# The reciprocal of a softmax's row sums issued one step later, and two subtractions of half a tile made one, in a hand-ordered attention pipeline

## The reference

```python
# q, k, v: (2, 8, 768, 64); centroids: (8, 16, 64)
q_assign = argmax(q_n @ c_n.T); k_assign = argmax(k_n @ c_n.T)
mask = q_assign[..., :, None] == k_assign[..., None, :]
scores = where(mask, scale * q @ k.T, -1e9)
attn = exp(scores - max(scores))
attn = attn / (sum(attn) + 1e-9)
x = (attn @ v)                      # as 1536 rows of 512
x = ((x @ w1) * (x @ w2)) @ w3 @ w_out
h = x @ w_in
out = (maximum(h, 0) + alpha * minimum(h, 0)) @ w_out2
```

## Time and profile before

| | |
|---|---|
| median of 3 runs | 774.82 us (771.75 to 774.99) |
| the profiled execution, its own time | 772.69 us |
| its span, first to last instruction | 770.9 us |
| mean granted TensorE clock | 0.998 |
| PE busy, PE weight loads busy | 750.2 us (97%), 644.9 us (84%) |
| DVE, ACT, POOL busy | 415.4 us (54%), 317.3 us (41%), 154.2 us (20%) |
| attention steps with turned tiles | from 74 to 317 us of the span |

### The profile page before, as it was taken

How to read it: one execution, slowest core, us unless ns; L and a number is a source line. 1 busy time by engine, 2 the same in 40 slices (tenths; PEclk the granted TensorE clock), 3 DMA queues, 4 the chain that set the end, 5 groups by cost and what they waited for, 6 DMA issues and landing times.

```text
span 770.9 us, 10682 instructions
## 1 busy us (share of the span) xinstructions
PE 750.2 (97%) x3810; PEld 644.9 (84%) x3810; DVE 415.4 (54%) x636; ACT 317.3 (41%) x627; POOL 154.2 (20%) x195
## 2 busy tenths in 40 slices
PE   5999999999999999899999999999999999999998
PEld 4888898898898897788888888888888888888886
DVE  4425989998899896642211153276333443434342
ACT  4325887888888786532211142242112101020112
POOL 2040544855747643210000000000000000000000
PEclk9999999999999999999999999999999999999999
DMA  9545375576666433320000021231000000010001
GB/s 293 159 111 132 75 166 123 124 157 134 133 140 143 95 77 86 102 83 1 0 1 1 0 82 57 80 102 63 0 1 33 23 1 1 1 54 1 1 0 55
DMA packets 64859, 55.74 MB, mean 72 GB/s; under 512 B 31520, under 2 KB 53040, under 8 KB 64816
## 3 DMA queue, kind: packets, MB, share of 16 engines
q1 hardware_dynamic: 64816, 55.16, 28.2%
HBM read 31.50 MB, written 3.19 MB: 45 GB/s over the span
## 4 chain that ended last, share of the span: by engine, by line
PE 76%; POOL 12%; issue 7%; DVE 3%; ACT 1%; POOLq 1%; DVEq 0%; ACTq 0%
PE slot L600 55%; PE acc L600 16%; PE slot L665 3%; POOL oh L510 1%; POOL v L484 1%; POOL v L480 1%; POOL c L502 1%; POOL c L503 1%; POOL xf L533 1%; PE acc L613 1%; DVE pl L1171 1%; DVE nm L1165 1%; PE slot L713 1%; POOL c L500 1%; POOL c L508 1%
## 5 line engine op out<-in xcount | busy, mean ns | idle before, releaser
L600 PE MATMUL slot<-xh,w 128*128 128x512 f32 x768 | 247.8, 389 | 0.0
L600 PEld LDWEIGHTS slot<-xh,w 128*128 128x128 f32 x768 | 144.3, 188 | 29.9
L600 PE MATMUL slot<-xl,w 128*128 128x512 f32 x384 | 149.5, 389 | 0.0
L1065 ACT CAST gh<-gf 128x512 fp32r<-128x512 f32 x48 | 29.9, 623 | 203.2 <-PE acc L600 186.0
L1165 DVE TENSOR_REDUCE nm<-slot 128x1 f32<-128x768 f32 x96 | 90.9, 947 | 19.3 <-PE slot L600 18.6
L1171 DVE TENSOR_TENSOR pl<-slot,ph 128x384 fp32r<-128x384 f32 x192 | 97.3, 547 | 5.8 <-ACT ph L939 5.5
L939 ACT CAST ph<-slot 128x384 fp32r<-128x384 f32 x192 | 83.7, 488 | 36.2 <-PE slot L665 35.8
L931 ACT ACTIVATE pf<-slot,nm 128x768 f32<-128x768 f32 x96 | 87.8, 915 | 14.6 <-DVE nm L1165 14.3
L665 PE MATMUL slot<-ident,pf 128*128 128x128 f32 x576 | 81.9, 276 | 6.8 <-DVE pl L1171 6.7
L600 PEld LDWEIGHTS slot<-xl,w 128*128 128x128 f32 x384 | 72.1, 188 | 14.9
L600 PE MATMUL slot<-k,q 96*128 96x384 f32 (+1 forms) x384 | 83.1, 337 | 0.0
(11 more groups left out here) (115 smaller groups left out, 1004.2 us busy)
## 6 DMA issues: line engine op xcount, KB each, us to landing
stage<-in_moe_w SPq DMA_DIRECT2D x16, 256.0 KB, 3.3
stage<-in_moe_w_in SPq DMA_DIRECT2D x16, 256.0 KB, 2.8
stage<-in_moe_w_out SPq DMA_DIRECT2D x16, 256.0 KB, 3.0
stage<-in_moe_w SPq DMA_DIRECT2D x6, 512.0 KB, 4.4
qk<-in_q SPq DMA_DIRECT2D x16, 192.0 KB, 4.0
qk<-in_k SPq DMA_DIRECT2D x16, 192.0 KB, 4.1
vn<-in_v SPq DMA_DIRECT2D x16, 192.0 KB, 4.1
q<-k SPq DMA_DIRECT2D x16, 192.0 KB, 3.7
```

What stands on the lines that cost most here:

```text
L600: return nc.tensor.matmul(o, a, b, start=start, stop=stop)
L1065: copy(gh[j % 2][:, :], gf[j % 2][:, :]).then_inc(gh_done, 1)
```

## The change

Two things are edited. The reciprocal (DVE), the write of its row and its spreading (SP) each go one step later (lags 2, 3, 4 become 3, 4, 5). And in the steps with m = 10, 11, 0, 1, 2, 3 the low part of the turned tile is one operation over both banks, 128x768, which waits for both high parts and then raises `pl_done` by two; in the other six steps it stays two operations of 128x384. The choice goes by m alone, so it also holds from step 82 on, where these steps have no operand work. Of 192 operations of 128x384, 96 become 48 of 128x768.

```diff
+OPERAND_STEPS = (10, 11, 0, 1, 2, 3)
...
-                j = inverted_now(c, last, 3)
+                j = inverted_now(c, last, 4)
                 if j is not None:
                     inverse_row(it, j)
-                j = inverted_now(c, last, 4)
+                j = inverted_now(c, last, 5)
                 if j is not None:
                     inverse_spread(it, j)
...
             def probabilities_lo(it, g):
+                if (g + LT) % 12 in OPERAND_STEPS:
+                    dve.wait_ge(ph_done, 2 * tile(it, g) + 2)
+                    tt_(pl[g % NPH][:, :, :], wide(turned_p), f32(ph[g % NPH][:, :, :]), ALU.subtract
+                        ).then_inc(pl_done, 2)
+                    return
                 for b in range(2):
                     dve.wait_ge(ph_done, 2 * tile(it, g) + b + 1)
                     tt_(pl[g % NPH][:, b, :], turned_p[:, b, 0:HS], f32(ph[g % NPH][:, b, :]), ALU.subtract
...
-                j = inverted_now(c, last, 2)
+                j = inverted_now(c, last, 3)
                 if j is not None:
                     inverse(it, j)
```

## The result

The changed kernel takes 774.50 us (median of 22 runs, 773.64 to 776.75), the kernel before 772.76 (22 runs). The ratio is 1.0021, 95% interval 1.0013 to 1.0029: slower by 1.6 us (1.0 to 2.2). That is inside the 0.5% called no change, but the sum had -0.2: small as it is, the difference goes the other way. That it came so near hides a step that failed, a loss that was not in the sum, and a gain that was not in it either. The profiled execution takes 774.49, of which its span is 772.7, against 772.69 and 770.9 before.

A forecast was written before the change was run, and what follows sets the result against it. PE, busy for 97% of the span, was taken as the bound. Gain 2.83 against losses 1.59 and 1.05 gave -0.2 us: 772.5 for the profiled execution, 774.6 as median; 80% range 769.5 to 779.5.

The forecast's parts named there:

- The reciprocal's stall goes: DVE's wait for POOL's row sums ends, so step 10's transposes lose their 1.04 us delay; T9 to T11 become 5.03.
- The rival in which the reciprocal still holds DVE: On DVE, the wait for POOL moves along to the pick: slower, 782.2 us; chance 0.05.
- The single low part's own time: DVE's 128x768 low-part operation takes 0.953 us, and 1.01 from its start to the released transposes.
- rival "dear": DVE's single low part costs 1.094 us, 0.14 more at 32 places: up to 780.6 us; chance 0.16.
- The ring: Turn to turn through the one buffer of turned tiles: 0.64 + 0.89 + 1.01 = 2.54 us, above PE's 2.39 with operand work.
- T81 to T88: Transposes of steps 81 to 88: 16.14 us becomes 17.73, from 5.03 and five turns of 2.54; loss 1.59.
- T94 to T97: Transposes of steps 94 to 97: 0.41 from later release and 0.64 from one longer turn; loss 1.05 us.
- The step that failed: SP's row write and spreading one step later were costed at nothing, since their readers come three steps later.
- The six periods: Transposes of m = 9 to m = 2, six times: 78.73 us becomes 75.90, 12.65 each; gain 2.83.
- The net: Whole kernel: -2.83 + 1.59 + 1.05 = -0.2 us, no change within 0.5%.
- The first rival: The single low part delays nothing and the reciprocal's gain stays: 8.6 us faster, 766.2 us; chance 0.09.
- The third rival: Reciprocal still holds DVE: 3.9 us lost in six periods, 2.5 in steps 82 to 88, 1.05 behind; 782.2; chance 0.05.

The follow-up runs named there:

- The splits: Against later reciprocal, masks first, two low-part operations: in six steps, either the first waits for both high parts (767.16 us) or both banks release at the end (768.36).
- the second experiment: Only the single low parts, against the kernel before; reciprocal, row and spreading stay at their old places: 780.72 us, ratio 1.0098.

## Why the prediction was right or wrong

- **The reciprocal's stall goes: right.** No wait is left at the reciprocal, T10 is not late, and T9 to T11 are 5.00 (5.03 forecast). The rival in which the reciprocal still holds DVE is refuted.
- **The single low part's own time: right.** 0.955 us for 0.953, and 1.01 from start to release. The rival "dear" is refuted; nothing about the operation is dear. DVE lost no time by it, two operations held it 0.93 and one 0.87 us.
- **The ring: right as a mechanism, mis-sized by 0.02 to 0.14.** The term for "its reader starts behind the pair of high parts" was 0.89, read where a reader had started 0.03 behind a single one; it measured 0.96, 0.10 behind the end. That belongs to the single operation: two operations that wait for both high parts start 0.03 behind, as had been read. In the last steps two turns of five start 1.07 behind the low part instead of 1.01. That makes the loss of T81 to T88 2.06 where 1.59 stood. The splits show that it takes both halves, the wait and the late release, to make the ring the bound.
- **T94 to T97: right** as far as it can be told. 0.89 lost, 1.05 forecast, in a stretch that moves by 0.4 from profile to profile. The ring in it is 2.62 where 2.54 was worked out.
- **The step that failed: "I cost these at nothing", on SP.** The sentence looked at the transfers that move and their readers. It did not look at the queue's other end: when DVE and PE get earlier by the 1.04 us of T10, a wait which had just been covered comes to light. The masks of the next pair stand in SP's queue behind a transfer that waits for POOL, and POOL had not become earlier. It takes 1.34 us of this change's 2.83, and 2.4 us (2.9 in medians) from what the later reciprocal alone could bring. The question that the prediction asked for DVE, what is late next, was not put to SP and PE's scores.
- **The six periods.** Of 2.83, 0.97 came; 1.34 went to the masks, 0.5 to rings of 2.62 and 2.68 in the last two periods. The 0.74 given back from T14 to T15 was not in the sum: the first step with cluster products is 2.97 to 3.00 long where it was 3.09 to 3.12, each time behind a step in which PE's loads had waited. No run tests why.
- **Not in the sum at all:** +0.9 us ahead of step 4, with the clock at 0.50 for 3 us; not shown to belong to the change.
- **The net.** -0.2 was forecast, +1.8 is in the profiles: +1.9 of missing gain, +0.4 more loss from T81 to T89, +0.9 ahead of step 4, against -0.7 given back at T15, -0.2 from T94 to T97 and -0.2 elsewhere. The range held it. That the net is small in both is a cancelling, not a confirmation of each term: 3.1 us of unforeseen loss stood against 1.1 of unforeseen gain. And that the forecast of 774.6 is so near the 774.50 measured is luck: it was counted from a median of three runs, 774.82, which lies 2.1 above the 772.76 of 22, and this error hides the 2.0 by which the net was wrong.
- **The first rival, 766.2,** had the price of the reciprocal right in size (8.6; measured 7.3, 6.2 to 8.4) for a kernel with the masks moved as well. Without that, the reciprocal alone brings 4.9. As a time the 766.2 is 2.1 too high, for the same reason as the forecast. The third rival's price, 7.45, for a stall that stays under the single low part, is what the second experiment measured (7.6).

The Trainium skill (Perfetto Trace Analysis, Optimizing Scalar/DVE Operations), which the prediction weighed, has its second half borne out: DVE at 54% busy was not saturated but made PE wait, and two pieces let work finish 8.6 us sooner than one (6.3 of it between T4 and T99). Of its saving for each grouped instruction, about 0.125 us, the rows show 0.06, 0.93 to 0.87.

## What to carry to other kernels

Where a buffer is single, price an edit by the ring through it, from one use to the next, and not by engine time: a merged operation adds its wait for the last producer at the front and its late release at the back, and each costs little as long as the ring stays shorter than the step. When a stall is removed, walk every queue that feeds the next steps, those of transfers above all, and ask which transfer stands behind a wait of an engine that has not become earlier. The best version was the removed stall with that queue put in order, and no merged operation at all.

## What the runs showed of the hardware

Every profile has three long stalls of PE: at about 18 us (2.13 to 2.54 us long), at step 95 (1.93 to 2.95) and at about 320 us (2.59). The granted TensorE clock fell for some 3 us at one or two of them and not at the others, and not by their length: at step 95 it fell with a stall of 1.93 and not with one of 2.95. With the later reciprocal alone it fell at step 95, behind the load that had waited 2.34 us (timeline, then windows of 1 us from it):

```profile
293.09 0.31 PEld L666 LDWEIGHTS slot<-ident,pf 128*128 128x128 f32 x3 [2.34 <-DVE pl L1177]
...
294.85 0.33 PEld L601 LDWEIGHTS acc<-pl,v 128*128 128x128 f32 x1
...
297.35 0.19 PEld L601 LDWEIGHTS acc<-pl,v 128*128 128x128 f32 x1
```

```profile
293.09:294.09 1.00, 1.00 (x7) 0.68 (x7) 1.00 (x2) 1.00 (x4) 0.00 (x0) 0.87 0.99 293
294.09:295.09 1.00, 1.00 (x4) 1.00 (x4) 0.99 (x3) 1.00 (x3) 0.00 (x0) 0.50 0.62 186
```

One weight load takes 0.33 us at 0.50 and 0.19 at 1.00. Kernels that had this fall (the later reciprocal alone, pairs in the last steps, the two later ones with two operations or with m = 2 and 3 alone) did not have the one at about 320 us, where the others, both kernels of the comparison among them, show a granted clock of 0.50 (1.6 us from T99 to the end). So kernels that differ in a few steps of attention, and runs of one kernel, have 1.0 to 1.7 us of half clock in different places. A difference as small as this case's 1.6 us has to be read by stretches: half of the 1.8 in the two profiled spans lies ahead of anything that was changed.
